# Second expert tile taken from the first six token tiles, with the last scatters and ranks moved behind it

## What is computed

```python
x = attention(q, k, v).reshape(1152, 512)          # 2 batches of 576 tokens
logits = x @ w_gate + modality_bias[modality_id]   # 8 experts
e_idx = argmax(logits); gate_w = softmax(logits)[e_idx]
for e in range(8):
    h = maximum(x[e_idx == e] @ w1[e], 0)          # 512 -> 1024
    out[e_idx == e] = gate_w * (h @ w2[e])         # 1024 -> 512
p = domain_probs / sum(domain_probs)
for e in range(4):
    out2 += p[:, e] * (maximum(out @ v1[e], 0) @ v2[e])
```

## Time and profile before

| what | value |
|---|---|
| time, median of 3 runs | 608.99 us (608.19 to 611.79) |
| the profiled execution | 613.12 us, its span 611.4 us |
| mean granted clock of PE | 0.993 |
| PE busy | 596.7 us (98%) |
| DVE, ACT, POOL busy | 349.6, 218.5, 299.4 us |
| DMA | 56.83 MB, mean 93 GB/s |

### The profile page before, as it was taken

The page is one execution under the profiler, slowest core; times in us unless marked ns, Lnnn a source line. Parts: engine busy times, 40 slices in busy tenths (PEclk is TensorE's granted clock), DMA queues, the critical chain, the costliest instruction groups (busy, mean ns, idle before and its releaser), DMA issues.

```text
span 611.4 us, 10240 instructions
## 1 busy us (share of the span) xinstructions
PE 596.7 (98%) x3597; PEld 523.3 (86%) x3598; DVE 349.6 (57%) x722; ACT 218.5 (36%) x543; POOL 299.4 (49%) x287
## 2 busy tenths in 40 slices
PE   7999799999999999999999999999999999999996
PEld 4898678887878889889899899899899899898895
DVE  6688776248983213684554554554654554554644
ACT  7667632358883322223122132132132131131230
POOL 5346411451000009539997846746657648546005
PEclk9899899999999999999999999999999999999999
DMA  8826546737971102002122112112012021120004
GB/s 197 218 90 226 190 144 249 231 101 288 316 272 19 34 18 70 0 1 70 70 69 71 35 34 70 33 38 69 6 63 69 1 68 34 34 69 0 0 0 154
DMA packets 25132, 56.83 MB, mean 93 GB/s; under 512 B 6800, under 2 KB 7824, under 8 KB 25104
## 3 DMA queue, kind: packets, MB, share of 16 engines
q1 hardware_dynamic: 16672, 32.06, 16.2%
q0 software_dynamic: 6848, 21.52, 10.7%
q10 hardware_dynamic: 1584, 2.88, 1.6%
HBM read 49.10 MB, written 7.36 MB: 92 GB/s over the span
## 4 chain that ended last, share of the span: by engine, by line
PE 82%; DMA 8%; DVE 3%; issue 2%; POOL 2%; SPq 1%; ACT 1%; DVEq 0%; POOLq 0%; ACTq 0%
PE banks L1699 30%; PE banks L1670 30%; PE banks L1605 7%; PE banks L1591 7%; DMA w_raw<-in_moe_w 3%; PE banks L1474 2%; DMA x_by_expert<-zero_row 2%; DMA kT<-in_kT 2%; POOL out L662 1%; DVE w_lo L969 1%; PE banks L1580 1%; PE banks L1502 1%; DMA x_tile<-x_by_expert 1%; PE banks L1568 1%; PE banks L1487 1%
## 5 line engine op out<-in xcount | busy, mean ns | idle before, releaser
L1321 DVE SCALAR_TENSOR_TENSOR acc<-banks,meta_s,acc 128x512 f32<-128x512 f32 x135 | 100.8, 748 | 62.2 <-PE banks L1699 62.1
L1699 PE MATMUL banks<-u_hi,h_hi 128*128 128x512 f32 x288 | 112.3, 390 | 0.0
L1699 PE MATMUL banks<-u_lo,h_hi 128*128 128x512 f32 x288 | 112.1, 389 | 0.0
L1699 PE MATMUL banks<-u_hi,h_lo 128*128 128x512 f32 x288 | 112.0, 389 | 0.0
L1368 DVE SCALAR_TENSOR_TENSOR h_lo<-banks,h_hi 128x288 fp32r<-128x288 f32 x112 | 50.9, 455 | 44.7 <-ACT h_hi L857 22.9
L1670 PE MATMUL banks<-x2T_hi,u_hi 128*128 128x288 f32 x232 | 68.4, 295 | 0.0
L1670 PE MATMUL banks<-x2T_lo,u_hi 128*128 128x288 f32 x232 | 68.4, 295 | 0.0
L1670 PE MATMUL banks<-x2T_hi,u_lo 128*128 128x288 f32 x232 | 68.3, 295 | 0.0
L845 ACT COPY part_p<-banks 128x288 f32<-128x288 f32 x28 | 11.2, 400 | 157.9 <-PE banks L1670 157.9
L1670 PE MATMUL banks<-t_hi,u_hi 128*128 128x288 f32 x224 | 66.2, 295 | 0.0
L1670 PE MATMUL banks<-t_lo,u_hi 128*128 128x288 f32 x224 | 66.0, 295 | 0.0
(11 more groups left out here) (242 smaller groups left out, 1223.5 us busy)
## 6 DMA issues: line engine op xcount, KB each, us to landing
w_raw<-in_moe_w SPq DMA_DIRECT2D x20, 1024.0 KB, 7.2
u_raw<-in_moe_w POOLq DMA_DIRECT2D x16, 512.0 KB, 3.9
u_raw<-in_moe_w POOLq DMA_DIRECT2D x16, 256.0 KB, 3.3
u_raw<-in_moe_w POOLq DMA_DIRECT2D x32, 128.0 KB, 2.9
x_tile<-x_by_expert ACTq DMA_DIRECT2D x11, 256.0 KB
x_by_expert<-zero_row SPq DMA_DIRECT2D x10, 256.0 KB, 2.8
qT<-in_qT SPq DMA_DIRECT2D x3, 576.0 KB, 6.3
kT<-in_kT SPq DMA_DIRECT2D x6, 288.0 KB, 8.8
```

What stands on the lines that cost most here:

```text
L1321: w.scalar_tensor_tensor(out=acc[:, t, :], in0=bank[Z_BANK[i]][:], scalar=meta_s[:, t, bass.ds(e + 1, 1)], in1=acc[:, t, :], op0=ALU.mult, ...
L1699: last = t_.matmul(bank[Z_BANK[i]][:], lhs[:, c, ts], rhs[page][:, c, :], start=c == 0 and k == 0, stop=c == 1 and k == 2)
```

## The change

Tile 1 is made of the tokens of t0 to t5 alone. PE also counts the tokens of six tiles behind the ranks of group 1 (`count_group`), and DVE works out where tile 1 ends and tile 2 starts (`place_second`, new semaphore `second_known`). SP writes 128 rows of zeros behind those rows before it reads x of tile 1. The ranks of group 2, its scatters and the count of all tokens move into tile 1; POOL waits for x of tile 1 before it scatters group 2. DVE finds the experts of group 2 behind tile 0's last `keep_ht`, and its table work starts behind the ranks. The table gets a second correction of row positions (`choice` column 7), since tiles 0 and 1 may both be partly filled. In tile 0 PE does HIGH of both halves, CROSS of both, then LOW of both. ACT cuts the first piece of w1 before it keeps the rows of t4, and the fourth before it keeps x of tile 0. In tile 1 x of tile 2 is flipped late in the second layer. Both halves of w2 are loaded behind x of tile 0. X of tile 3 is loaded by SP, not ACT.

```diff
@@ sync
             load_w1(0, w1_early)
             load_w1(1, w1_in)
-            load_w2(0, w2_early)
             sp.wait_ge(x_first_known, 3)
...
             sp.dma_start(x_tile[:], xb[bass.ds(x0, P), :]).then_inc(xt_in, 16)
+            load_w2(0, w2_early)
             load_w2(1, w2_in)
             x1 = sp.value_load(x_first[0:1, 1:2], min_val=0, max_val=(E - 1) * ROWS + P)
+            sp.wait_ge(second_known, 2)
+            tail = sp.value_load(x_first[0:1, 4:5], min_val=0, max_val=(E - 1) * ROWS + N)
+            sp.dma_start(xb[bass.ds(tail, P), :], zero_row[:]).then_inc(filled_a, 16)
+            x2 = sp.value_load(x_first[0:1, 2:3], min_val=0, max_val=(E - 1) * ROWS + 2 * P)
+            sp.wait_ge(filled_a, 32)
+            sp.wait_ge(scattered, 16 * (GROUPS[1][1] - GROUPS[1][0]))
+            sp.wait_ge(xt_flipped, 1)
+            sp.dma_start(x_tile[:], xb[bass.ds(x1, P), :]).then_inc(xt_in, 16)
             sp.wait_ge(fill_known, 1)
             tail = sp.value_load(fill_at[0:1, bass.ds(expert, 1)], min_val=0, max_val=(E - 1) * ROWS + N)
             sp.dma_start(xb[bass.ds(tail, P), :], zero_row[:]).then_inc(filled_a, 16)
-            sp.wait_ge(filled_a, 32)
+            sp.wait_ge(filled_a, 48)
             sp.wait_ge(scattered, 16 * (NT - GROUPS[0][1]))
-            sp.wait_ge(xt_flipped, 1)
-            sp.dma_start(x_tile[:], xb[bass.ds(x1, P), :]).then_inc(xt_in, 16)
-            sp.wait_ge(x2_known, 1)
-            x2 = sp.value_load(x_first[0:1, 2:3], min_val=0, max_val=(E - 1) * ROWS + 2 * P)
             sp.wait_ge(xt_flipped, 2)
             sp.dma_start(x_tile[:], xb[bass.ds(x2, P), :]).then_inc(xt_in, 16)
...
             sp.wait_ge(table_ready, 1)
+            x3 = sp.value_load(x_at[0:1, 4:5], min_val=0, max_val=E * ROWS - P)
+            sp.wait_ge(filled, 16 * E)
+            sp.wait_ge(xt_flipped, 3)
+            sp.dma_start(x_tile[:], xb[bass.ds(x3, P), :]).then_inc(xt_in, 16)
@@ gpsimd
             put_in_order()
-            pool.wait_ge(xt_in, 16)
             for g_ in (1, 2):
                 t0, t1 = GROUPS[g_]
+                pool.wait_ge(xt_in, 16 * g_)
                 pool.wait_ge(slot_ready, g_ + 1)
@@ scalar
-            keep_rows(LOOP_TILES)
             act.wait_ge(w1_early, 16)
             cut_w1(0)
+            keep_rows(LOOP_TILES)
             keep_prob(STEPS - 2)
...
             keep_rows(GROUPS[2][0])
+            cut_w1(3)
+            keep_xt(0)
             keep_rows(GROUPS[2][0] + 1)
-            keep_xt(0)
-            cut_w1(3)
...
             keep_ht(1, 0)
             keep_h(1, 1)
+            keep_ht(1, 1)
             keep_xt(2)
-            keep_ht(1, 1)
+            keep_y(1)
             act.wait_ge(table_ready, 1)
-            act.wait_ge(filled, 16 * E)
-            load_x(act.value_load(x_at[0:1, 4:5], min_val=0, max_val=E * ROWS - P))
             n_tiles = act.value_load(table[0:1, 1, 1:2], min_val=EARLY + 1, max_val=MAXT)
-            keep_y(1)
@@ vector
+            def place_second(count):
+
+                dve.wait_ge(order_known, 1)
+                step(w.tensor_tensor(n_e0[:], count, is_e0[:], ALU.mult))
+                step(w.reduce_sum(choice[:, 6:7], n_e0[:], axis=AX.X))
+                w.tensor_tensor(x_first[:, 4:5], choice[:, 2:3], choice[:, 6:7], ALU.add).then_inc(second_known, 1)
+                step(w.tensor_scalar(choice[:, 4:5], choice[:, 3:4], float(P), choice[:, 6:7], ALU.add, ALU.min))
+                w.tensor_tensor(x_first[:, 2:3], choice[:, 2:3], choice[:, 4:5], ALU.add).then_inc(second_known, 1)
...
             split_w1(0, 0)
             keep_xt(0)
+            split_w1(0, 1)
             add_logits(t8)
-            dve.wait_ge(logit_read, NT - LOOP_TILES)
-            find_experts(slice(*GROUPS[2]))
-            split_w1(0, 1)
             split_w1(0, 2)
-            dve.wait_ge(rank_done, 2)
-            keep_ranks(slice(*GROUPS[2]), bank[7][:, 0:(GROUPS[2][1] - GROUPS[2][0]) * E])
-            find_slots(slice(*GROUPS[2]))
             split_w1(0, 3)
-            dve.wait_ge(counted, 1)
-            step(w.tensor_copy(n_tok[:], bank[6][:, 0:E]))
-            w.tensor_tensor(fill_at[:], n_tok[:], e_rows[:], ALU.add).then_inc(fill_known, 1)
+            t0, t1 = GROUPS[1]
+            place_second(bank[5][:, (t1 - t0) * E:(t1 - t0 + 1) * E])
...
+                w.tensor_scalar(tile_pad[:], tile_no[:], 2.0, choice[:, 7:8], ALU.is_ge, ALU.mult).then_inc(vstep, 1)
...
+                w.tensor_tensor(base_at[:], base_at[:], tile_pad[:], ALU.subtract).then_inc(vstep, 1)
...
             keep_ht(0, 1)
+            dve.wait_ge(logit_read, NT - LOOP_TILES)
+            find_experts(slice(*GROUPS[2]))
             keep_xt(1)
+            find_last()
             count_tiles()
             find_offsets()
+            keep_ht(1, 0)
             make_table()
+            keep_ht(1, 1)
             dve.wait_ge(x2_hi_kept, 1)
+            dve.wait_ge(scattered, 16 * (NT - GROUPS[0][1]))
             w.tensor_tensor(x2T_lo[:, :, 0:P], bank[6][:].rearrange("p (c t) -> p c t", c=DC),
                             x2T_hi[:, :, 0:P].bitcast(FP32), ALU.subtract).then_inc(x2_lo_kept, 1)
             mark_tiles()
-            keep_ht(1, 0)
             keep_xt(2)
             sum_tiles()
-            keep_ht(1, 1)
             place_tiles()
@@ tensor
-            rank_group(t0, t1, bank[5][:, 0:(t1 - t0) * E]).then_inc(rank_done, 1)
+            rank_group(t0, t1, bank[5][:, 0:(t1 - t0) * E])
+            count_group(t1, bank[5][:, (t1 - t0) * E:(t1 - t0 + 1) * E]).then_inc(rank_done, 1)
             rows_and_logits(t7)
...
             x_w1(0, 0, (HIGH,))
             x_w1(0, 1, (HIGH,))
-            rank_last()
             pe.wait_ge(xt_kept, 1)
-            x_w1(0, 0, (CROSS, LOW)).then_inc(h_done, 1)
+            x_w1(0, 0, (CROSS,))
             x_w1(0, 1, (CROSS,))
+            x_w1(0, 0, (LOW,)).then_inc(h_done, 1)
+            x_w1(0, 1, (LOW,)).then_inc(h_done, 1)
             pe.wait_ge(x_kept_a, kept_by_act(NT - 1))
             flip_h(0, 0)
+            pe.wait_ge(second_known, 1)
+            second_layer(0, 0, lambda: flip_x(1))
+            pe.wait_ge(xt_hi_kept, 2)
+            x_w1(0, 0, (HIGH,))
+            rank_last()
+            pe.wait_ge(xt_kept, 2)
+            x_w1(0, 0, (CROSS, LOW)).then_inc(h_done, 1)
+            flip_y(1)
+            x_w1(0, 1, (HIGH, CROSS))
+            flip_h(1, 0)
             x_w1(0, 1, (LOW,)).then_inc(h_done, 1)
-            second_layer(0, 0, lambda: flip_x(1))
-            whole_tile(1, 0)
+            second_layer(1, 0, lambda: flip_x(2))
```

More of the change, by code:

```diff
@@ L1086, in _, with find_last @@
             keep_xt(0)
+            split_w1(0, 1)
             add_logits(t8)
[L1088 to L1090 removed]
             split_w1(0, 2)
[L1092 to L1094 removed]
             split_w1(0, 3)
[L1096 to L1098 removed]
+            t0, t1 = GROUPS[1]
+            place_second(bank[5][:, (t1 - t0) * E:(t1 - t0 + 1) * E])
+            def find_last():
+                t0, t1 = GROUPS[2]
+                at = (t1 - t0) * E
+                dve.wait_ge(rank_done, 2)
+                keep_ranks(slice(t0, t1), bank[7][:, 0:at])
+                find_slots(slice(t0, t1))
+                step(w.tensor_copy(n_tok[:], bank[7][:, at:at + E]))
+                w.tensor_tensor(fill_at[:], n_tok[:], e_rows[:], ALU.add).then_inc(fill_known, 1)
             def split_w2(r, c):
@@ L1135, in count_tiles @@
                  .then_inc(lmax_known, 1)
[L1136 to L1139 removed]
+                step(w.tensor_scalar(early_n[:], is_e0[:], choice[:, 4:5], None, ALU.mult))
+                w.tensor_scalar(choice[:, 7:8], choice[:, 3:4], choice[:, 4:5], float(P), ALU.subtract, ALU.add).then_inc(vstep, 1)
+                st.next()
                 fill_others()
@@ L1561, in rank_last @@
                 pe.wait_ge(slot_ready, 2)
-                rank_group(t0, t1, bank[7][:, 0:(t1 - t0) * E]).then_inc(rank_done, 1)
-                count_group(t1, bank[6][:, 0:E]).then_inc(counted, 1)
+                rank_group(t0, t1, bank[7][:, 0:(t1 - t0) * E])
+                count_group(t1, bank[7][:, (t1 - t0) * E:(t1 - t0 + 1) * E]).then_inc(rank_done, 1)
             def flip_x(j):
```

29 lines of the change are left out of this document (10 added, 19 removed).

## The result

The changed kernel is slower, by half a per cent. Its median is 612.35 us (607.93 to 613.97, 11 runs), that of the kernel before on the same chip 608.55 us (606.60 to 611.79, 11 runs). The ratio is 1.0058, 95% interval 1.0038 to 1.0078, which is 3.5 us more where the forecast had 3.0 us less. A second comparison gave 1.0084 (1.0063 to 1.0105). The profiled execution took 612.35 us, its span 610.6 us, its mean granted clock 0.995.

What follows compares the result with a forecast made beforehand. PE was taken to bound: what it gains before about 105 us counts one for one. Gains 2.6, 1.5 and 0.4, less 0.4 (ranks) and 1.1 (tables), give 3.0 us off the 608.99 us median: 606.0 us, range 603.9 to 609.2.

Steps and rivals of the forecast that it cites:

- middle stretch: From PE's product for token tile 7 to its first product of expert tile 3; forecast 44.34 us, 47.36 before.
- Step 1: x of tile 0: with w2's first half behind it, x arrives at 64.0 and PE's whole 2.25 us wait goes.
- Rival A: No gain at x of tile 0: third scatter still takes 7 us to land; 608.6 us, chance 0.12.
- Step 2: First layer of tile 0: 1.1 us stall gone, about 1.0 us idle behind flip_h, second layer 4.1 us earlier, at 74.35.
- rival C: New zero fill for x of tile 1 takes 7.3 us because w2's loads still flow; 609.9 us, chance 0.07.
- Rival D: New idle times in tiles 0 to 2 drop PE's clock to half once, costing 1.7 us; 607.7 us, chance 0.1.
- Step 3: x of tile 1: new fill in time with 0.5 us slack, tile 1 starts at 80.9, 4.5 us earlier; 0.4 us booked.
- Step 4: Tile 1: last group's ranks add 0.49 us, x of tile 2 stays hidden; tile 2 starts at 94.3, 4.1 us earlier.
- Step 5: Table work: table_ready at 98.1, hardly earlier; PE stalls 1.0 us for x of tile 3, giving back 1.1 us.
- Rival B: Tables do not bind: DVE's chain is 1.0 us shorter, so 1.1 us is not given back; 604.9 us, chance 0.12.
- slow stretch: PE at half clock near 67 to 70 us, after its 2.25 us wait; about 0.35 us net booked as removed.

Runs made afterwards that it cites:

- e2: Changed kernel with three of ACT's copies for tile 0 moved ahead of its wait for w2's second half and two cuts; 606.97 us, ratio 0.9979.
- e3: Kernel before with only both halves of w2 loaded behind x of tile 0; 607.33 us, ratio 0.9987.
- k7: Kernel before with both halves of w2 behind x of tile 0 and ACT's copies of h ahead of its wait for w2's second half; 605.56 us, ratio 0.9969.
- e4: e2 with ACT's tile 2 written out ahead of its loop, its first copy of h before the table wait and register loads; 606.21 us, ratio 0.9978.

## Why the prediction was wrong

I forecast 606.0 us (603.9 to 609.2) and the median was 612.35. Against the forecast's own middle stretch (44.34 us) the change came out 5.3 us longer (49.66), and the table above says where: 0.34 us up to the flip of x0, 2.64 from there to the second layer, 1.38 in the second layer, 0.12 in tile 1 and 0.84 in tile 2. The stretch before that I took as the base was moreover 0.7 us long.

**Step 1, right, but one term mis-sized.** The wait fell from 2.25 to 0.58 us, and with w2 behind x the fill was no longer what ended last. The third scatter was: the chain has it at 5.51 us, issued at 55.52, where I took 3.6 (57.6 to 61.2) by dividing what was left by 0.38 MB/us. That rate did not hold to the end. Windows of the changed kernel:

```profile
57.00:58.00 1.00, 1.00 (x8) 1.00 (x9) 0.93 (x4) 1.00 (x2) 0.68 (x2) 1.00 1.02 404
58.00:59.00 1.00, 1.00 (x20) 0.89 (x20) 0.43 (x3) 0.77 (x2) 1.00 (x2) 1.00 0.39 152
59.00:60.00 1.00, 1.00 (x14) 0.72 (x11) 0.86 (x3) 0.92 (x3) 0.83 (x4) 1.00 0.07 29
60.00:61.00 1.00, 1.00 (x10) 0.87 (x11) 0.90 (x5) 1.00 (x3) 0.73 (x3) 1.00 0.03 12
```

For two of its 5.5 us the scatter was a tail of 29 and 12 GB/s at a DMA share of 0.07 and 0.03, about one of 16 engines. PE came to the flip that much sooner too (attention was 2 us shorter in this trace), so that x was 1.7 us later against PE than forecast; 1.4 us of slack in the forecast took most of it. Rival A, no gain at x0, did not happen.

**Step 2 is the step that failed.** Its own items came true: HIGH began 3.58 us behind token tile 7's product (forecast 3.4), no wait for `w_lo`, all low products done by 71.4, an uncovered flip of 0.72 us where I had 1.0. But I followed ACT only up to `keep_xt(0)`. Between that and `keep_h(0, 0)` its queue has four cuts of w2, and I never set the arrival of w2 beside them, although the change moves w2's first half from ahead of x to behind it, and although rival C says that those loads may flow until 70. They did: issued at 61.69 and 62.16, the second landed at 71.38. Two cuts behind that (1.99 us) put h at 73.3 where PE wanted it at 71.36. Before the change, all cuts of w2 were done well ahead of h:

```profile
76.34 0.60 ACT L725 ACTIVATE h_tile<-banks 128x512 f32<-128x512 f32 x1 [1.96 <-PE banks L1591]
```

ACT had been idle for 1.96 us there, and PE took h at 77.08, 13.1 us behind token tile 7. In the changed kernel PE asked for h at 9.3 us, and the last load of w2 was issued at 0.1 us: that left 9.2 us for its landing, the two cuts and the copy of h. Landing and cuts alone took 11.2, with the copy 11.9, and the 2.7 us between are the stall. The order of the queue and ACT's slack of 1.96 us stood in the trace of before and in the two kernels, the landing time of 9.2 us did not; e2 showed that this queue was the cause.

**Rival D came true as a consequence.** I gave the clock 0.1 and 1.7 us, on the strength of new idle times of 0.4, 1.0 and 1.0 us. None of those did it; the stall that I had missed did, with 1.41 us (1.98 in the second trace). In the first trace the half clock came behind 2.68 us of stall and 0.63 us of work, within the 0.72 us that follow; in the second it came within the stall of 2.81 us itself. In before a stall of 2.25 us had it, one of 2.74 us did not. The Trainium skill (TensorE: Matmul & The Clock Gate, What's actually happening) has the slow state as the default, which activity lifts. That the clock falls only behind idle time agrees with it; these traces do not say which stall lets it fall.

**Step 3, right.** SP's new fill (71.01) was down before the read (73.97), and x of tile 1 was there at once (81.95 without a wait). Rival C, the late fill, did not happen, though its premise, w2 flowing until 71, did: it hit another reader. But e3 and k7 show that this step had nothing to win either: the 0.4 us that I booked was before's 0.29 us.

**Step 4, right.** Tile 1 took 13.52 us (forecast 13.4), with the ranks at 84.26, x of tile 2 there without a wait.

**Step 5, right in kind, wrong in the reader.** The last table value came 17.5 us after T1 (forecast 17.2). I expected PE to wait 1.0 us for x of tile 3, and wrote that ACT's h of tile 2 "ends at the same place, inside this stall". It ended later: behind the table ACT loads its registers for 2.35 us (100.86 to 103.21), not 1.5, and h was the wait, 1.55 us. The 0.8 us for x of tile 3 were there behind it, as e4 showed when it took the first away. T2 to T3 took 14.86 us, forecast 14.02. The table was ready at 100.8, beyond the 99 that I had named as a sign of being wrong: mostly because tile 1 began 2.4 us late (83.32 against 80.9). Rival B, tables that do not bind, did not happen.

**The base.** One execution of before, 613.12 us, was 4.5 us of span above a second one. That moved neither the sign nor the forecast much, since the sum was put on the median; but 0.35 us for the slow stretch and 0.4 us at x1 were read off that one trace.
